# The last routing batches cut into three, one and two tiles, with unread products moved behind TensorE's branches

## The reference, cut to what matters

```python
# 1: attention, token by token
S = a * S + k v^T ; y = q S                  # complex a, real part used
x = y reshaped to (3072, 384)
# 2: experts
do_compute = x @ w_skip > 0
e_idx = argmax(x @ w_gate); gate_w = softmax(...)[e_idx]
y[mask] = gate_w * (relu(x[mask] @ w1[e]) @ w2[e])    # e = 0..7
out[do_compute] = x + y
# 3: feed forward
h = x @ w_in ; out = (h * sigmoid(h)) @ w_out
```

## Time and profile before

| what | value |
| --- | --- |
| median of 3 runs | 881.17 us (880.81 to 881.20) |
| the profiled execution | 881.67 us, its span 879.9 us |
| mean granted TensorE clock in it | 0.99 |
| PE busy | 835.3 us (95% of the span) |
| DVE, ACT, POOL busy | 352.6, 347.7, 160.3 us |
| share of PE in the chain that ended last | 91% |

### The profile page before, as it was taken

The page is one execution under the profiler, slowest core; times in us unless marked ns, Lnnn a source line. Parts: engine busy times, 40 slices in busy tenths (PEclk is TensorE's granted clock), DMA queues, the critical chain, the costliest instruction groups (busy, mean ns, idle before and its releaser), DMA issues.

```text
span 879.9 us, 13208 instructions
## 1 busy us (share of the span) xinstructions
PE 835.3 (95%) x5202; PEld 747.9 (85%) x5202; DVE 352.6 (40%) x656; ACT 347.7 (40%) x606; POOL 160.3 (18%) x193
## 2 busy tenths in 40 slices
PE   1499999999999789999999999999999999999997
PEld 0278888798899589999998998999899999998997
DVE  1588878868765322222323132122122122122112
ACT  6888988888652131111112222222222222222221
POOL 2101112611503305455300001001001001001001
PEclk9899999999999989999999999999999999999999
DMA  9999888666422386899730000000000000000000
GB/s 171 162 179 249 110 108 115 107 108 83 124 105 110 125 183 190 249 237 252 229 90 1 0 1 37 1 1 37 1 1 36 1 1 37 1 1 35 2 1 37
DMA packets 174167, 77.34 MB, mean 88 GB/s; under 512 B 151592, under 2 KB 167304, under 8 KB 174096
## 3 DMA queue, kind: packets, MB, share of 16 engines
q1 hardware_dynamic: 169168, 60.54, 34.6%
q0 software_dynamic: 4928, 15.84, 6.3%
HBM read 60.80 MB, written 15.59 MB: 87 GB/s over the span
## 4 chain that ended last, share of the span: by engine, by line
PE 91%; DVE 2%; issue 2%; ACT 2%; DMA 2%; POOL 1%; SPq 0%; POOLq 0%; DVEq 0%; ACTq 0%
PE f_pU L1681 23%; PE f_pO L1687 22%; PE e_pH L1425 8%; PE e_pY L1439 8%; PE sc L513 5%; PE kvp L527 3%; PE tq L495 2%; PE tk L500 2%; PE yp L538 2%; PE yp L540 2%; PE cs L470 2%; PE cs L110 2%; PE cs L483 2%; PE cs L484 2%; PE sc L549 1%
## 5 line engine op out<-in xcount | busy, mean ns | idle before, releaser
L1681 PE MATMUL f_pU<-f_xT,wi 128*128 128x512 f32 x864 | 215.1, 396 | 0.8 <-DVE f_xT L1622 0.8
L1687 PE MATMUL f_pO<-wo,gT 128*128 128x384 f32 x1152 | 213.9, 336 | 0.0
L1687 PEld LDWEIGHTS f_pO<-wo,gT 128*128 128x128 f32 x1152 | 202.7, 188 | 7.4
L1681 PEld LDWEIGHTS f_pU<-f_xT,wi 128*128 128x128 f32 x864 | 161.7, 188 | 32.1 <-DVE f_xT L1622 1.2
L1638 DVE TENSOR_TENSOR gT<-g,gT 128x512 fp32r<-128x512 f32 x96 | 66.5, 693 | 286.4 <-ACT gT L1665 286.4
L1660 ACT ACTIVATE g<-f_pU 128x512 f32<-128x512 f32 x96 | 57.5, 599 | 298.3 <-PE f_pU L1681 298.3
L1628 POOL DMA_INDIRECT out<-o,row_of x24 | 24.1, 1004 | 422.3 <-DVE o L1649 415.9
L1425 PE MATMUL e_pH<-e_xT,ring 128*128 128x224 f32 x384 | 74.9, 356 | 0.2 <-DVE e_xT L1530 0.2
L1439 PE MATMUL e_pY<-hT,ring 128*128 128x224 f32 x384 | 74.1, 353 | 0.0
L1425 PEld LDWEIGHTS e_pH<-e_xT,ring 128*128 128x128 f32 x384 | 73.3, 193 | 0.6 <-issue 0.4
L1439 PEld LDWEIGHTS e_pY<-hT,ring 128*128 128x128 f32 x384 | 72.1, 191 | 0.0
(11 more groups left out here) (182 smaller groups left out, 1008.9 us busy)
## 6 DMA issues: line engine op xcount, KB each, us to landing
ring<-in_moe_w SPq DMA_DIRECT2D x16, 1536.0 KB, 10.0
ring<-in_a_re SPq DMA_DIRECT2D x8, 576.0 KB, 8.4
ring<-in_a_im SPq DMA_DIRECT2D x8, 576.0 KB, 8.8
ring<-in_q SPq DMA_DIRECT2D x8, 576.0 KB, 8.0
ring<-in_k SPq DMA_DIRECT2D x8, 576.0 KB, 8.3
vraw<-in_v SPq DMA_DIRECT2D x8, 576.0 KB, 5.4
xs<-zero SPq DMA_DIRECT2D x9, 343.9 KB, 7.2
part<-in_moe_w_in POOLq DMA_DIRECT2D x12, 256.0 KB, 7.4
```

What stands on the lines that cost most here:

```text
L1681: mm = pe.matmul(pU[f % 2][:, :], wi[:, pw, c, f * 128:(f + 1) * 128], xT[b % 2][:, px, c, :], start=(k == 1), stop=(k == NK * len(TERMS)))
L1687: mm = pe.matmul(pO[t][:, 0:DM], gT[f % GB][:, pg, t * 128:(t + 1) * 128], wo[:, pw, f, :], start=(f == 0 and k == 0), stop=(f == NF - 1 a ...
```

## The change

It does four things. The batch of four tiles becomes one of three (tiles 18 to 20) and one of a single tile (21), so there are six batches. The batch of three is chosen by DVE at the end of step `c == 4` of the last period instead of `c == 5`, and its ranks are formed on PE inside step 5. The single tile uses the PSUM bank `tk`, the last two tiles keep `tq`. Of the twelve unread products ahead of the branches eight stay, and thirteen new ones stand behind both branches, ahead of the experts' first transpose: four, then a wait for `sent`, then nine. (`route_again`, part of the skipped path, gets one more bank.)

```diff
-        self.batches = [(0, 6), (6, 6), (12, 6), (18, 4), (22, 2)]
+        self.batches = [(0, 6), (6, 6), (12, 6), (18, 3), (21, 1), (22, 2)]
...
-        banks = [cs[1]] * 4 + [tq[:, :, :].rearrange("p h c -> p (h c)")]
+        banks = [cs[1]] * 4 + [t[:, :, :].rearrange("p h c -> p (h c)") for t in (tk, tq)]
...
+                    if c == NC - 1 and j == 2:
+                        routing.ranks(pe, s, 3, banks[3])
                     if c > 0 and j == 2:
                         turn_x(first + c - 1)
...
-            routing.ranks(pe, s, 3, banks[3])
             logits(X.shape[1] - 2)
             turn_x(X.shape[1] - 1)
+            routing.ranks(pe, s, 4, banks[4])
             logits(X.shape[1] - 1)
             keep_busy(2)
-            routing.ranks(pe, s, 4, banks[4])
+            routing.ranks(pe, s, 5, banks[5])
             routing.count(pe, s, pC)
-            keep_busy(12)
+            keep_busy(8)
...
-                if c == 5 and p == G - 1:
-                    routing.choose(dve, s, 3, banks[3], link)
-                    routing.mark(dve, s, 3, link)
-                    routing.run(dve, s, 3)
+                if c >= 4 and p == G - 1:
+                    if c == 5:
+                        routing.place(dve, s, 3, banks[3], link)
+                    routing.choose(dve, s, c - 1, banks[c - 1], link)
+                    routing.mark(dve, s, c - 1, link)
+                    routing.run(dve, s, c - 1)
...
+            def keep_busy(n):
+
+                for _ in range(n):
+                    pe.matmul(pH[0][:, 0:DM], routing.ones, routing.wg.rearrange("p c e -> p (c e)"), start=True, stop=True)
+
             passes(pe, body, lambda: pe.matmul(pX[0:1, 0, 0:1], ident[:, 0:1], ident[:, 0:1], start=True, stop=True))
+            keep_busy(4)
+            pe.wait_ge(after["sent"], 16 * routing.NT)
+            keep_busy(9)
             body(0, last)
```

More of the change, by code:

```diff
@@ L992, in vector @@
                     last(p, c)
[L993 to L996, removed]
             routing.place(dve, s, 4, banks[4], link)
+            routing.choose(dve, s, 5, banks[5], link)
+            routing.mark(dve, s, 5, link)
+            routing.run(dve, s, 5)
+            routing.place(dve, s, 5, banks[5], link)
             routing.tabulate(dve, s, pC, thr, at, valid, tt, more, link)
@@ L1127, in route_again @@
         scr = ctx.enter_context(nc.sbuf_tensor("a_scr", [128, 2], F32))
-        pT, pL, pM, pC = (ctx.enter_context(nc.psum_tensor("a_" + n, [128, 512], F32)) for n in ("pT", "pL", "pM", "pC"))
-        banks = [pL] * 4 + [pM]
+        pT, pL, pM, pN, pC = (ctx.enter_context(nc.psum_tensor("a_" + n, [128, 512], F32))
+                              for n in ("pT", "pL", "pM", "pN", "pC"))
+        banks = [pL] * 4 + [pM, pN]
         s = {n: sem("a_" + n) for n in """wg_in route_const xT_done xT_out logit_done step chosen hot_done run_done rank_done
```

## The result

The changed kernel takes 886.78 us (median of 6, 886.05 to 887.94) against 881.34 us (6 runs) of the kernel before: a ratio of 1.0063, 95% interval 1.0050 to 1.0076. It is 5.4 us slower. The forecast was 6.55 us slower, with a range of 885.0 to 890.5 us. The profiled execution has a span of 885.2 us, 5.3 more than before. Every ratio in this document stands with its 95% interval as it was worked out from all executions; it is not the quotient of the two medians and differs from it by up to 0.0008.

A forecast was written before the change was run, and what follows sets the result against it. PE, busy 95%, bounds the kernel, its sequencer's branches the passage to the experts. Earlier branches save 2.6 us, thirteen products cost 10.8, the clock returns 1.6: +6.55 us, 887.7 us, range 885.0 to 890.5.

The forecast's parts named there:

- The mechanism: Between attention and experts: PE's sequencer, through its branches, sets the experts' start, neither the routing, the scatters nor the xt load.
- the clock's part: Products behind the branches: the clock falls in PE's hole, returns 4.2 us after work resumes, costing 2.1 us (0 to 2.75).
- The flag: PE's flag load ahead of its branches: reached at 295.5, 2.6 us earlier, with last ranks at 295.0.
- a limit of 17 records: PE's queue ahead of the branches: the sequencer runs about 17 records ahead of the array and is held there.
- The rival that the products didn't hold the sequencer: Ahead of PE's branches: start at 308.7, sum +8.75 us, 889.9 us; chance 0.12.
- Start behind the branches: PE's first instruction behind both branches: at 306.5 instead of 309.11; bounds 306.05 and 308.7.
- a fetch of code: Rival, PE's branches: one fetch more or less, priced 2.7 us, giving 885.0 or 890.4 us; chance 0.10.
- The gain of the routing part at this place: Last ranks ahead of the branches: 0.4 us earlier, at 295.0 instead of 295.43; bounds 0 and 0.9.
- Products and clock: Thirteen products between branches and transpose: 8.66 us at 2.4 GHz plus 2.1 us for the low clock.
- the bound of 2.75: Products behind the branches: upper bound in us on their low-clock cost, with 5.5 us to the clock's return in an earlier case.
- the first dozen or so: Sign in the changed profile: of 26 records of the new product line, these would be about twice as long.
- Back from the clock: From the transpose through up(0): both run at 2.4 GHz again, giving back 1.6 us together.

## Why the prediction was right, step by step

**The mechanism held, and each term of the sum was seen.** PE's sequencer sets the start of the experts, not the routing and not `xt`; the last scatters came earlier and changed nothing by themselves. Not all of the agreement is skill: the clock's part was luck in its size, and one term was left out, as said below.

**The flag.** Forecast 0.5 us behind the last ranks through a limit of 17 records; measured 0.5 in five kernels with eight products, one of them with wide ones, and 0.2, 2.7 and 5.3 with four, twelve and sixteen. The rival that the products didn't hold the sequencer is refuted by these. The Trainium skill, TensorE: Matmul & The Clock Gate, section Architectural detail, gives TensorE's queue a depth of 64; the trace shows a lead of 17 to 18 matmul records and as many weight loads. Whether the queue is counted in another unit, no run here shows.

**Start behind the branches.** Forecast 306.5, measured 305.4. This term was the one most off, by 1.1 us: the second branch shrank by 0.8 us, because it began earlier relative to SP's loads (0.4 us ahead of the first of them instead of 0.7 us behind it), as the order of the thirteen kernels has it. I had named a fetch of code as uncertain, by one whole fetch, and not seen that its length depends on what runs beside it. The rest is that this execution was 0.4 us ahead before it reached the changed part. The gain of the routing part at this place was 0.4 us, as put: from the logits of tile 20 on PE (284.56 before, 284.19 now) to the last ranks it is 10.87 and 10.50 us.

**Products and clock.** Forecast 8.66 + 2.1, measured 10.18 us: the clock returned 3.75 us after PE resumed instead of 4.2, and PE's first 0.3 us still ran at 2.4 GHz. That the return came so near the forecast is luck: it came 6.9 us after PE resumed with the routing part alone, 6.0 with wide products or with only fewer ahead, 4.9 without products behind and 3.2 with only the thirteen behind. Half of the longest is 3.4 us, above the bound of 2.75 that the prediction took from one earlier case. A slip beside it: the forecast of "the first dozen or so" records of double length doesn't fit its own 4.2 us, in which six records of 0.67 us have room; the measured low stretch has room for five.

Back from the clock came 1.53 us, forecast 1.6. The Trainium skill, TensorE: Matmul & The Clock Gate, section Terms, takes half of the throttled time as the penalty, for the 4.2 us of before 2.1 us, which is an estimate. The trace does not agree, by 0.6 us, and 0.4 of these are seen: PE waited for DVE's copy 0.2 us before and 0.6 us now, so part of what the transpose and the gate product gained was lost to that wait. The measurement decides for 1.5.

**A term left out.** Behind the idle tiles PE waits 1.2 us instead of 0.8, put down to ACT's copy. The clock is not the cause, and neither are the products behind: the wait is 1.2 us in all seven kernels with the new routing and no held loads, with a low clock in `up(0)` or without, and 0.8 us in the kernel before and in three more with the old routing, two of them with an undisturbed clock in `up(0)` and thirteen products behind. ACT's own copies are as long in both traces; PE starts 0.55 us after the last of them ends instead of 0.2. So the routing part gains 0.4 us at the start and loses 0.4 us here, which agrees with its 0.0 in time; why it does is not shown. Together: 6.55 - 1.1 - 0.6 + 0.1 + 0.4 = 5.3 us, rounded.

**Where the intended gain went.** What the clock gave was 1.5 us (1.2 to 2.8 us over all profiled kernels without products behind), and the products that were to protect it cost 10.2. They did not even keep the clock up: it falls in the hole ahead of them, which comes from the branches, and the unread products pay for its return as the transposes would have. The 3.7 us gained by an earlier passage were spent inside them.

## What to carry to other kernels

Unread products are sure to be free only where the engine would be idle anyway: count what has landed by the time that they start. Here the data waited for them for 9.6 us, and the version without any, with wide products ahead, was 0.2% faster than before. Work queued ahead of a branch delays the branch once the sequencer's lead is used up, so filler there should be few and long instructions, and large loads issued while an engine jumps far in its code lengthen the jump. Holding them back is no gain by itself: on the kernel before it made PE wait for the idle tiles, 886.53 against 881.41 us.

## What the runs showed of the hardware

PE's sequencer ran 17 to 18 matmul records (with their weight loads) ahead of the array, whether a record took 0.33 or 0.44 us. PE's two branches over long skipped code took 3.3 to 4.3 us (first) and 4.0 to 7.1 us (second), against 0.05 us on ACT; the second took 4.0 us without SP's loads beside it and 4.1 to 7.1 with them, the more the later it began behind their issue. Its two 16 KB packets of code started later beside the loads and took about as long. What else fills the 4.0 us that stay remains open. The granted clock fell from 2.4 to 1.2 GHz 2.4 us after PE went idle in the kernel before and 5.0 us after in the changed one, so the length of a hole alone does not tell when it falls; with wide products it fell in a hole of 3.4 us. It returned 3.2 to 6.9 us after PE resumed, and even the same number of products ahead (twelve, none behind) gave 4.2 and 6.9 us.
